# A recurrent-attention stage whose inputs come turned from the host, whose output is made turned and turned back, with the router's logits one round nearer

## What is computed

```
# attention, per batch and head, token by token
y[t]  = r[t] @ (state + (u * k[t]) outer v[t])
state = w[:, None] * state + k[t] outer v[t]
# x[b, s] = y of the 8 heads side by side (384 values)
logits = x @ w_gate ; gate = sigmoid(x @ w_local)
e = argmax(logits) where s == 0 or gate < 0.5, else the expert of the token before
x = softmax(logits)[e] * (relu(x @ w1[e]) @ w2[e])
# MLP
out = x + relu(norm(x) * g_ln @ w_ch1) @ w_ch2
```

## Time and profile before

| | us |
|---|---|
| median of 3 runs (lowest, highest) | 432.27 (431.03, 433.51) |
| the profiled execution's own time | 430.16 |
| its span, from the first to the last instruction | 428.4 |
| TensorE busy | 389.9 |
| DVE, ACT, POOL busy | 230.9, 139.5, 127.8 |
| mean granted clock of TensorE, share of 2.4 GHz | 0.949 |

### The profile page before, as it was taken

The page is one execution under the profiler, slowest core; times in us unless marked ns, Lnnn a source line. Parts: engine busy times, 40 slices in busy tenths (PEclk is TensorE's granted clock), DMA queues, the critical chain, the costliest instruction groups (busy, mean ns, idle before and its releaser), DMA issues.

```text
span 428.4 us, 7278 instructions
## 1 busy us (share of the span) xinstructions
PE 389.9 (91%) x2640; PEld 369.6 (86%) x2640; DVE 230.9 (54%) x424; ACT 139.5 (33%) x283; POOL 127.8 (30%) x128
## 2 busy tenths in 40 slices
PE   6899999965059999999999999899999999999993
PEld 6799999864049999999999999788998899988993
DVE  5797779965406473663745769586203652133110
ACT  0434645320007254382553735452002220022000
POOL 5595563704605235053250521300100001100010
PEclk9999999965559999999999999999999999999998
DMA  7999984073544959477584270410010001000001
GB/s 114 154 252 222 241 222 56 20 252 116 187 129 134 291 193 361 173 279 263 195 319 157 103 260 1 131 57 2 18 38 18 0 2 37 27 12 2 18 20 37
DMA packets 62249, 54.76 MB, mean 128 GB/s; under 512 B 41216, under 2 KB 56960, under 8 KB 62208
## 3 DMA queue, kind: packets, MB, share of 16 engines
q1 hardware_dynamic: 47744, 19.58, 20.1%
q10 hardware_dynamic: 12032, 26.74, 17.9%
q0 software_dynamic: 2432, 7.92, 4.9%
HBM read 43.13 MB, written 11.10 MB: 127 GB/s over the span
## 4 chain that ended last, share of the span: by engine, by line
PE 79%; DVE 9%; DMA 4%; ACT 2%; issue 2%; SPq 1%; POOLq 1%; POOL 0%; ACTq 0%; DVEq 0%
PE bank L1199 21%; PE bank L1201 21%; PE bank L1200 21%; PE bank L1161 3%; PE bank L1158 2%; PE bank L1146 2%; PE bank L1136 2%; DVE split L366 2%; PE bank L1112 2%; PE bank L1170 1%; PE bank L1194 1%; DMA vn<-in_v 1%; DMA kn<-in_k 1%; ACT dv L612 1%; PE bank L1125 1%
## 5 line engine op out<-in xcount | busy, mean ns | idle before, releaser
L361 ACT CAST split<-raw 128x1024 fp32r<-128x1024 f32 (+1 forms) x60 | 59.2, 1004 | 0.0
L1199 PE MATMUL bank<-xT,split 128*128 128x256 f32 x192 | 55.4, 288 | 2.1 <-DVE xT L900 2.1
L1200 PE MATMUL bank<-xT,split 128*128 128x256 f32 x192 | 55.2, 287 | 0.0
L1201 PE MATMUL bank<-xT,split 128*128 128x256 f32 x192 | 55.1, 287 | 0.0
L366 DVE TENSOR_TENSOR split<-raw,split 128x1024 fp32r<-128x1024 f32 (+1 forms) x40 | 52.7, 1331 | 1.8 <-ACT split L361 1.7
L591 POOL DMA_INDIRECT out<-orow,cpos x12 | 11.7, 974 | 132.8 <-DVE orow L1029 132.8
L1199 PE MATMUL bank<-split,h2T 128*128 128x384 f32 x144 | 48.7, 338 | 0.0
L1201 PE MATMUL bank<-split,h2T 128*128 128x384 f32 x144 | 48.2, 335 | 0.0
L1200 PE MATMUL bank<-split,h2T 128*128 128x384 f32 x144 | 48.2, 334 | 0.0
L366 POOL TENSOR_TENSOR split<-raw,split 128x1024 fp32r<-128x1024 f32 (+1 forms) x20 | 45.8, 2310 | 6.0 <-ACT split L361 3.4
L703 ACT ACTIVATE h2T<-bank 128x512 fp32r<-128x512 f32 x36 | 21.5, 598 | 72.8 <-PE bank L1201 71.7
(11 more groups left out here) (164 smaller groups left out, 754.7 us busy)
## 6 DMA issues: line engine op xcount, KB each, us to landing
raw<-in_w ACTq DMA_DIRECT2D x14, 1536.0 KB, 7.3
raw<-in_w_ch ACTq DMA_DIRECT2D x2, 2304.0 KB, 8.9
xsort<-zeros SPq DMA_DIRECT2D x8, 388.0 KB, 3.2
X<-xsort SPq DMA_DIRECT2D x8, 388.0 KB, 5.4
ysort<-yrow POOLq DMA_DIRECT2D x8, 388.0 KB, 7.0
raw<-in_w SPq DMA_DIRECT2D x2, 1536.0 KB, 8.5
X<-ysort SPq DMA_DIRECT2D x3, 776.0 KB, 5.4
rn<-in_r SPq DMA_DIRECT2D x12, 192.0 KB, 5.2
```

Of the source, the lines that this page charges most:

```text
L361: act.copy(hi, src).then_inc(s_hi, 1)
L1199: pe.matmul(dst, stationary[0], moving[0], start=first, stop=False)
L1200: pe.matmul(dst, stationary[0], moving[1], start=False, stop=False)
L1201: return pe.matmul(dst, stationary[1], moving[0], start=False, stop=last)
```

## The change

The host lays out r and k already turned and padded (`rkT`, 4 KB for each partition and chunk), k and r a second time with tokens on partitions (`rows_kr`, without padding), v by chunks, and all weights as one run for each partition. In the kernel:

- TensorE's 8 transposes of r and k are gone. DVE scales only k (`scale_k`, L825), from SBUF and one chunk ahead; POOL scales r (`scale_r`, L525), from SBUF. `rk`, `rku`, `ks` and `ub` lose their padding, and `state` and `stsum` have 192 columns in place of 384, with each head in its own half of the partitions.
- y is made turned, in bank 0: the weights are `state` (64 rows, 48 columns) and `vn` (128 rows, 48 columns), the moving operands `rT` and `sc` (128 columns), and the result of a head goes to its half of the partitions. ACT copies it to `yTs`, TensorE turns it back into bank 4 (4 transposes), and DVE adds `dv` to it. The state is advanced by 8 products of 64 weight columns and 48 moving columns.
- There are two rounds behind the first instead of three: in round i TensorE makes the scores of chunk i, y of chunk i-1, and the logits of chunk i-2. v has a ring of 4. ACT makes `dv` in two parts of 4 heads, before and after the copy of y. `choose(0)` comes in round 10, `places(0)` stands inside round 12, DVE's pieces of the split in rounds 9, 11, 12 and 13, and POOL's in rounds 10 and 11.

```diff
-    need(sp, s_rkt, i - RING + 1)
-    need(sp, s_ks, i - RING + 1)
-    sp.dma_start(rn[q][:, :, 0:Dh], r[b, :, rows, :].rearrange("h t d -> t h d")).then_inc(s_r[q], 16)
-    sp.dma_start(kn[q][:, :, 0:Dh], k[b, :, rows, :].rearrange("h t d -> t h d")).then_inc(s_k[q], 16)
+    need(sp, s_rT, i - RING + 1)
+    need(sp, s_kT, i - RING + 1)
+    sp.dma_start(tin[q][:], rkT[i]).then_inc(s_t[q], 16)
...
+    sp.dma_start(kr[q][:], rows_kr[i]).then_inc(s_kr[q], 16)
...
+def scale_r(i):
+    pool.wait_ge(s_t[i % RING], 16 * (i // RING + 1))
+    need(pool, s_yp, i - 2)
+    pool.tensor_tensor(rT[i % 3][:], tin[i % RING][:, 0], wp, ALU.mult).then_inc(s_rT, 1)
...
+def scale_k(i):
+    dve.wait_ge(s_t[i % RING], 16 * (i // RING + 1))
+    need(dve, s_scp, i - B + 1)
+    dve.tensor_tensor(kT[i % B][:], tin[i % RING][:, 1], wn, ALU.mult).then_inc(s_kT, 1)
...
+    if 0 <= j < NT:                                  # ACT, j = i - 1
+        act.wait_ge(s_dg, j + 1)
...
+        dg_times_v(j, range(H // 2))
+        act.wait_ge(s_yp, j + 1)
+        need(act, s_bk, j)
+        act.copy(yTs[:].rearrange("p n t -> p (n t)"), bank[0][:]).then_inc(s_ye, 1)
+    if i >= 2:
+        act.wait_ge(s_lp, i - 1)
+        act.copy(LG[:, i - 2, :], bank[7][:, D:D + E + 1]).then_inc(s_lg, 1)
+    if 0 <= j < NT:
+        dg_times_v(j, range(H // 2, H)).then_inc(s_dvp, 1)
...
-        pe.matmul(bank[4][:, n * 2 * Dh:(n + 1) * 2 * Dh], rT[j % 3][:, n, :], state[b][:, n, :], start=True, stop=False)
-        for h in range(2):
-            last = pe.matmul(bank[4][:, (2 * n + h) * Dh:(2 * n + h + 1) * Dh], sc[b][:, h, n, :],
-                             vn[j % RING][:, 2 * n + h, :], start=False, stop=(h == 1))
+        for h in range(2):                           # TensorE, y of chunk j = i - 1, for each n
+            pe.matmul(bank[0][halves[h], n * P:(n + 1) * P], state[b][h * HALF:(h + 1) * HALF, n, :],
+                      rT[j % 3][h * HALF:(h + 1) * HALF, n, :], start=True, stop=False)
+        for h in range(2):
+            last = pe.matmul(bank[0][halves[h], n * P:(n + 1) * P], vn[j % VRING][:, 2 * n + h, :], sc[b][:, h, n, :],
+                             start=False, stop=True)
...
+        pe.wait_ge(s_ye, j + 1)
+        need(pe, s_x, j)
+        for n in range(NP):
+            last = pe.transpose(bank[4][:, n * P:(n + 1) * P], yTs[:, n, :], ident[:])
+        last.then_inc(s_bk, 1)
```

More of the change, by code:

```diff
@@ L542, in _ @@
                     pool.wait_ge(s_yp, j + 1)
[L543 to L544 removed]
+                    pool.tensor_tensor(state[b][:], stsum[b][:], wst[:], ALU.mult).then_inc(s_st, 1)
                 if i == 2:
                     late_constants()
[L547 to L549 removed]
+                if NT - B <= i < NT:
+                    split_lo(pool, 0, i - NT + B)
+            assert B == POOL_CK
             for ph in range(NPH):
@@ L860, in _ @@
                     dve.wait_ge(s_rku, i + 1)
-                    dve.tensor_reduce(dg[b][:], rku[:], AX_X, ALU.add).then_inc(s_dg, 1)
-            places(0)
+                    dve.tensor_reduce(dg[b][:], rku[:].rearrange("p (h d) -> p h d", h=H), AX_X, ALU.add).then_inc(s_dg, 1)
+                if i == ROUTED[0]:
+                    carry_on(0)
+                if i == ROUTED[0] + 1:
+                    chosen(0)
+                if i in LATE_LO:
+                    split_lo(dve, 0, POOL_CK + LATE_LO.index(i))
+            assert len(LATE_LO) == CK - POOL_CK
             choose(1)
@@ new lines, in _ @@
+                    pe.wait_ge(s_rT, i + 1)
+                    pe.wait_ge(s_kT, i + 1)
+                    need(pe, s_sc, 2 * i)
+                    for n in range(NP):
+                        for h in range(2):
+                            q = slice(h * HALF, (h + 1) * HALF)
+                            last = pe.matmul(bank[2 + h][:, n * P:(n + 1) * P], kT[b][q, n, :], rT[i % 3][q, n, :],
+                                             start=True, stop=True)
+                    last.then_inc(s_scp, 1)
@@ L1135, in _ @@
                     for n in range(NP):
-                        last = pe.matmul(bank[5][:, n * 2 * Dh:(n + 1) * 2 * Dh], ks[b][:, n, :],
-                                         vn[j % RING][:, 2 * n:2 * n + 2, :].rearrange("p h d -> p (h d)"), start=True, stop=True)
+                        for h in range(2):
+                            q = slice(h * HALF, (h + 1) * HALF)
+                            last = pe.matmul(bank[5][q, n * Dh:(n + 1) * Dh], ks[b][:, n, q], vn[j % VRING][:, 2 * n + h, :],
+                                             start=True, stop=True)
@@ L1138, in _ @@
                     last.then_inc(s_u, 1)
                 if 0 <= j < NT:
-                    b = j % B
-                    pe.wait_ge(s_kT, j + 1)
-                    need(pe, s_sc, 2 * j)
-                    for n in range(NP):
-                        for h in range(2):
-                            q = slice(h * HALF, (h + 1) * HALF)
-                            last = pe.matmul(bank[2 + h][:, n * P:(n + 1) * P], kT[b][q, n, :], rT[j % 3][q, n, :],
-                                             start=True, stop=True)
```

300 lines of the change are left out of this document (139 added, 161 removed).

## The result

The changed kernel takes 426.94 us, the median of 4 runs (423.79 to 427.67), beside 432.89 us for the kernel before in the same session (431.03 to 434.13): a ratio of 0.986, with an interval of 0.982 to 0.989. It is faster by 1.4%. The forecast was 418 us, so the direction was right and the gain, 6 us, less than half of the 14.4 that were forecast. The profiled execution took 423.79 us, for a span of 422.2.

A forecast was written before the change was run, and what follows sets the result against it. TensorE's groups bound the rounds and experts, DVE leads the tail, POOL's scatters chain routing. -7.2 - 5.5 + 1.0 - 2.7 = -14.4 from 430.16 gives 415.8; with the median's 2.1 more, 418 us, range 408 to 429.

The forecast's parts named there:

- A: Start, up to the scores of chunk 2: these start at 16.2 instead of 23.4 us, -7.2 us.
- Chunk 1's need its own load (near 9) and POOL's scaling behind one `rk`, near 10.5: Start: the scores of chunk 1 wait for their load and POOL's scaling, and start near 10.5 us.
- Rival 4: Start: first transfers 5 times as large, so the early start brings nothing; -3 us, total 422; chance 0.07.
- B: Eight rounds, scores of chunk 2 to those of chunk 10: 5.95 instead of 6.64 us each, -5.5 us.
- the sum 1.09 + 0.35 + 2.7 + 0.64 + 0.7 + 0.46: TensorE's round: scores, turned X, y, logits, state and turning y back; 5.94 us, taken as 5.95.
- Rival 1: Rounds: halves with v run in sequence, shape changes cost in full; y 3.98, round 7.2, total 429 us; chance 0.14.
- Rival 2: Rounds: another engine's loop or the transfers hold the round at 6.6 us, gain nearly 0, total 423; chance 0.14.
- C: Tail, scores of chunk 10 to last logits copied: 26.7 instead of 25.7 us, +1.0 us.
- D: Routing, last logits to first expert product: last scatter ends 11.3 instead of 14.0 us behind the logits, -2.7 us.
- What lies behind is the same: Routing, after the last scatter: the way to the first expert product is unchanged.

The follow-up runs named there:

- e10: Changed kernel with chunk 1's turned r and k loaded ahead of chunk 0's rows, and POOL scaling that r before its first `rk`; 425.44 us, ratio 0.985.
- e12: Changed kernel with y's products grouped, 30 dummy products at the start, DVE's last split piece in round 12 and the second turned load first; 414.27 us, ratio 0.958.
- e9: Changed kernel with y's products grouped by shape, 30 dummy products at the start and DVE's last split piece in round 12; 415.30 us, ratio 0.961.
- e4: Changed kernel with 30 dummy products on TensorE behind the scores of chunk 0; 424.82 us, ratio 0.987.
- e5: Changed kernel with DVE's last split piece in round 12 instead of 13, so the third expert's load starts earlier; 425.07 us, ratio 0.983.
- e1: Changed kernel with y's products grouped: all 8 with the state first, then all 8 with v; 417.43 us, ratio 0.969.
- e2: Changed kernel with y's products grouped and the state's 8 products moved between y and the logits; 418.26 us, ratio 0.968.
- The control: The changed kernel run once more, unaltered; 426.06 us, ratio 0.988.
- e3: Changed kernel with the third expert's weights load issued right behind the load of the first expert's rows; 426.72 us, ratio 0.989.
- e11: Changed kernel with the third expert's weights load issued only once the first expert's rows have landed; 430.37 us, ratio 0.996.
- e7: Changed kernel with y not turned (tokens on partitions, no copy or turning back) and 30 dummy products at the start; 459.78 us, ratio 1.062.

## Why the prediction was right in direction and wrong in size

**The start (A, 3.1 us of the miss): the step "Chunk 1's need its own load (near 9) and POOL's scaling behind one `rk`, near 10.5" failed.** The scores of chunk 0 came at 8.02 (8.5 forecast). The second turned load landed at 10.7, 7.24 us after its issue at 3.44. I had given each transfer the rate that a queue had in the mean, and one after another; from 8 to 12 us the engines moved 376 to 416 GB/s with a share of 1.01 to 1.04, so they were full, and 576 KB stood between this load and the first. Putting it first lets it land 4.0 us sooner, but brings the scores of chunk 1 on by only 0.9 us (e10), and those of chunk 2 by 1.25 where the clock is held (e12 beside e9). What holds chunk 1 then is a second thing that the step left out: DVE masks the scores of chunk 0 before it scales k of chunk 1, so that they could not have started at 10.5 even with the load in time. The third, which the prediction did not have at all, is that TensorE idles for 3.4 us and runs at its 1.2 GHz level behind that: the scores of chunk 2 come 1.4 us sooner in the one profile in which this was filled (e4), and 2.1 sooner in the one in which the clock stayed up by itself (e5). With the load and the clock mended they start at 16.2. Rival 4 (A is -3) came near the number, in part for its reason, the size of the transfers.

**The round (B, 3.2 us of the miss): the step that failed is the sum 1.09 + 0.35 + 2.7 + 0.64 + 0.7 + 0.46, which charges changes of shape inside y alone.** The price of a change, 0.13 from the earlier trace rows, was right (0.135 in e1). But X, the logits and the turning back each follow a group of another shape now, and each is 0.13 longer: 0.39 in all. y is 2.83 for 2.7, the state 0.60 for 0.7. Together 0.13 + 0.39 - 0.10 = 0.42, eight times 3.3 us, which is the whole miss of B. That y came so near was luck: a pass is 0.055 where I took 0.068 (the 0.068 of the scores had a change in it), which is 0.4 less for 32 passes, and the eight changes cost 1.08 in full where I charged 0.52, which is 0.56 more. Rival 1 joined two causes; the changes are real, and halves that run one after the other are not. The Trainium skill ("TensorEngine Tiling (Array Packing)", Key Properties) says that changing the tiling mode drains the engine, and that tiles of one mode work in parallel; the runs agree with both, at 0.135 us a change and 0.055 us a pass. That it is a drain which takes the 0.135 us the traces do not show.

**Nothing else bounds the round.** DVE, POOL and ACT wait for TensorE in the changed kernel, and TensorE for none of them from 20 to 76 us. Rival 2 was wrong for this kernel, and e2 shows where it begins, in the order of the products that e2 has: at 5.6 us.

**The tail (C)** was right in the profile that was taken first, +1.2 for +1.0, with the clock's fall in it. The control has +2.1 for the same kernel, so the near hit was in part luck. It goes with the clock: in the five profiles with turned y in which it stays at 0.50 until the experts (the control, e2, e3, e5, e11) C is 27.5 to 27.8 us, in those in which it comes back for a while (the changed kernel, e1, e4, e9, e10, e12) 26.2 to 26.8.

**Routing (D): the scatters were right, and what stood beside them was missed.** The first starts at 88.87, 8.1 us before the last logits are copied (7 forecast), and the last 10.0 us behind them. The step "What lies behind is the same" failed (2.1 us of the miss): with DVE's last piece in round 13 and an earlier end of routing, the third expert's load came upon the scatters and made the last one 2.5 us longer (1.4 in the control). e3, e5 and e11 show that it goes with the load. But half of D's miss stays without it: D is then 20.7 to 20.9 us (e3, e5, e11), where 19.7 were forecast. The trace gives the idle time of TensorE before its first product on the rows as 13.28 us (e11), 13.36 (e3), 13.35 (e9), 13.53 (e5) and 13.81 (e12), and there it starts only 0.8 to 1.6 us after the rows have landed (0.35 in the control, with 13.60); where that idle time is 14.0 us or more (e1, e2, e4, e10 and the changed kernel) it starts as they land. So something besides the rows seems to hold it for some 13.3 us behind its last small product of routing. The program has a candidate: before TensorE waits for the rows it waits for `s_meta` and reads ten counts from `meta`, which DVE writes behind the last places. DVE's last such write ends 8.0 us before the first product in the changed kernel, 6.9 to 7.0 us before it in e3, e9 and e11, and in no run less than 6.9. No run changed these reads, so it stays open. In the changed kernel at most 1.1 us (14.34 - 13.28) are to be won by the rows' landing sooner, in the control 0.3.

**The median.** The changed kernel's profiled execution was the fastest of its four by 2.5 us, with a mean clock of 0.952 where the others have 0.938 to 0.942; the spread goes with the clock. By its medians the change is worth 6.0 us, by its profiles 6.4.

## What to carry to other kernels

Price every change of the array's shape (64 to 128 rows, whole to half columns) on whatever group follows it, here 0.13 us each, and group the products by shape first; here that was worth more than twice as much as all the other edits together (the median of e12 is 3.2 us below that of e1, and that of e1 8.6 below the control's; these ran on three chips, and the ratios say the same: 0.958, 0.969, 0.988). When large loads take the place of small ones, look at what stands ahead of the second one in its queue, what the engine that uses it does first in its own order, and what the wait does to TensorE's clock. When a piece of work is moved to a later round, follow the load that it releases to what that load then runs beside. And profile the same kernel twice before a difference of 1 us in one stretch is believed.

## What the runs showed of the hardware

- TensorE's clock fell to its 1.2 GHz level and stayed there (0.50 from 20 to 60 us) in a kernel whose TensorE records there have no gap (e7), where y moves 48 columns against 128 columns of weights instead of 128 against 48; filling part of the wait ahead of it did not help.
- Two products with weights of 48 columns in the two column halves and 128 rows cost 0.055 us a pass, as much as those of 64 rows side by side, and a change between the two shapes 0.135 us (e1 beside the changed kernel).
- The last indirect transfer of 128 rows, which lands in 2.6 to 2.9 us when no large load is under way (e3, e5, e11), takes 4.0 to 5.1 us when a 3 MB load that fills the DMA engines (398 GB/s) has held up those ahead of it (the changed kernel and the control).
- Between the end of its routing products and its first product on the experts' rows TensorE never had less than 13.28 us, even with its data there for 1.6 us.
- TensorE's clock fell behind a wait of 3.4 us at the start in one execution and stayed at 1.00 behind one of 2.74 us in another (e5) and of 2.08 us in a third (e9, behind its dummy products); behind one of 2.5 us it fell (e10).
